# Recurrent attention and experts on one core: probabilities first on VectorE, idle products, a unit's scores split, loads in another order, two units a slot later

## What is computed

```
for t in range(S):
    m_new = maximum(f[t] + m, i[t])
    C = exp(f[t] + m - m_new) * C + exp(i[t] - m_new) * outer(v[t], k[t])
    n = exp(f[t] + m - m_new) * n + exp(i[t] - m_new) * k[t]
    y[t] = sigmoid(o[t]) * (C @ q[t]) / maximum(abs(n . q[t]), 1)
x = y as (1536, 320);  p = domain_probs / sum(domain_probs)
out = sum over 4 experts e of p[:, e] * (relu(x @ w1[e]) @ w2[e])       # w1 320x1024, w2 1024x320
```

## Time and profile before

| | us |
|---|---|
| median of 3 runs | 417.99 |
| the three runs | 418.11, 417.26, 417.99 |
| the profiled execution | 418.08 |
| its span, first to last instruction | 416.4 |
| busy: TensorE / VectorE / ScalarE / GpSimd | 411.6 / 180.6 / 158.5 / 152.3 |

### The profile page before, as it was taken

How to read it: one execution, slowest core, us unless ns; L and a number is a source line. 1 busy time by engine, 2 the same in 40 slices (tenths; PEclk the granted TensorE clock), 3 DMA queues, 4 the chain that set the end, 5 groups by cost and what they waited for, 6 DMA issues and landing times.

```text
span 416.4 us, 7050 instructions
## 1 busy us (share of the span) xinstructions
PE 411.6 (99%) x2710; PEld 398.3 (96%) x2710; DVE 180.6 (43%) x372; ACT 158.5 (38%) x329; POOL 152.3 (37%) x189
## 2 busy tenths in 40 slices
PE   8999999999999999999999999999999999999997
PEld 8899999999999999999999999999999999999996
DVE  5875796646555556446223232323113132311313
ACT  4575477745355653514112431144211333211111
POOL 4865735595174925304011660065100453000000
PEclk9999999999999999999999999999999999999999
DMA  7999939678513845300000231024200000000101
GB/s 269 272 283 394 369 100 354 226 256 290 189 37 131 303 132 193 122 2 0 2 0 2 85 129 67 0 71 139 71 0 2 0 0 2 34 0 2 63 0 65
DMA packets 16899, 48.45 MB, mean 116 GB/s; under 512 B 1921, under 2 KB 8594, under 8 KB 15714
## 3 DMA queue, kind: packets, MB, share of 16 engines
q1 hardware_dynamic: 16290, 46.60, 31.9%
q10 hardware_dynamic: 576, 1.40, 1.0%
HBM read 45.94 MB, written 2.05 MB: 115 GB/s over the span
## 4 chain that ended last, share of the span: by engine, by line
PE 98%; DVE 1%; issue 0%; DVEq 0%
PE hid_ps L1076 42%; PE acc_ps L1095 37%; PE out_ps L1032 5%; PE score_ps L1095 3%; PE acc_ps L1076 2%; PE out_ps L1039 2%; PE score_ps L976 2%; PE add_ps L1011 1%; PE hid_ps L925 1%; PE score_ps L971 1%; PE acc_ps L1032 0%; PE out_ps L1051 0%; PE out_ps L1052 0%; PE out_ps L1053 0%; PE score_ps L989 0%
## 5 line engine op out<-in xcount | busy, mean ns | idle before, releaser
L810 DVE SCALAR_TENSOR_TENSOR h_lo<-hid_ps,h_hi 128x384 fp32r<-128x384 f32 (+2 forms) x120 | 68.0, 567 | 219.7 <-ACT h_hi L587 219.6
L587 ACT ACTIVATE h_hi<-hid_ps 128x384 fp32r<-128x384 f32 (+2 forms) x120 | 59.6, 497 | 231.9 <-PE hid_ps L1076 231.8
L1095 PE MATMUL acc_ps<-w_hi,h_hi 128*128 128x320 f32 x352 | 110.2, 313 | 0.0
L1095 PE MATMUL acc_ps<-w_hi,h_lo 128*128 128x320 f32 x352 | 108.8, 309 | 0.0
L1095 PE MATMUL acc_ps<-w_lo,h_hi 128*128 128x320 f32 x352 | 108.4, 308 | 0.0
L1076 PE MATMUL hid_ps<-xt_hi,w_hi 128*128 128x384 f32 (+2 forms) x360 | 104.1, 343 | 0.1
L1076 PE MATMUL hid_ps<-xt_hi,w_lo 128*128 128x384 f32 (+2 forms) x360 | 103.7, 342 | 0.0
L441 POOL TENSOR_TENSOR w_lo<-w_raw,w_hi 128x384 fp32r<-128x384 f32 x56 | 58.9, 1054 | 114.5 <-ACT w_hi L573 114.5
L1076 PEld LDWEIGHTS hid_ps<-xt_hi,w_lo 128*128 128x128 f32 x360 | 65.4, 189 | 4.3
L1095 PEld LDWEIGHTS acc_ps<-w_hi,h_hi 128*128 128x128 f32 x352 | 66.3, 188 | 1.3
L1095 PEld LDWEIGHTS acc_ps<-w_lo,h_hi 128*128 128x128 f32 x352 | 66.3, 188 | 1.3
(11 more groups left out here) (172 smaller groups left out, 371.9 us busy)
## 6 DMA issues: line engine op xcount, KB each, us to landing
w_raw<-in_w_b SPq DMA_DIRECT2D x27, 704.0 KB, 4.3
raw<-in_qk_s SPq DMA_DIRECT2D x8, 1024.0 KB
g_all<-g_dram SPq DMA_DIRECT2D x10, 512.0 KB, 6.1
kv<-in_kv_n SPq DMA_DIRECT2D x12, 352.0 KB, 5.9
q_pack<-in_q_p SPq DMA_DIRECT2D x10, 192.0 KB, 6.1
out_y<-y_acc SPq DMA_DIRECT2D x12, 160.0 KB, 1.8
carry<-g_dram SPq DMA_DIRECT2D x30, 60.0 KB
y_acc<-in_o_n SPq DMA_DIRECT2D x1, 1280.0 KB, 12.3
```

What stands on the lines that cost most here:

```text
L587: nc.scalar.activation(h_hi[:, M % RING, 0:cols], hid_bank(M)[:, 0:cols], ACT.Relu).then_inc(hid_hi, 1)
L810: nc.vector.scalar_tensor_tensor(h_lo[:, M % RING, 0:cols], hid_bank(M)[:, 0:cols], 0.0, h_hi[:, M % RING, 0:cols].bitcast(fp32), ALU.max, ...
L1095: last = nc.tensor.matmul(acc_ps[t][:, 0:DM], x, w, start=(f == 0 and i == 0), stop=(f == NF - 1 and i == 2))
```

## The change

- Start, VectorE: `unit_maxima` moves ahead of all `probs`; `unit_steps` comes over from GpSimd and stands with `gate_scan(1)` ahead of `gate_x(0)`. The copy of the first key weights goes to ScalarE (`first_keys`), and the turned keys go to `hid_ps[0]` instead of `acc_ps[2]`.
- Start, TensorE: `move_ends` and `move_starts` come ahead of exponents and scores, and `keep_clock(3)` comes ahead of `outputs(0)`. `outputs(1)` waits for `w_tok`, not for `key_tok`.
- Start, ScalarE: pair 3 is issued and block 2 is split between the two `xt_high`; the scores of unit 3 are issued and the gates of tiles 2 and 3 opened between `relu(0)` and `relu(1)`.
- `NS` goes from 4 to 3: the fourth unit's (k = 3) scores take the split form, with casts in slots 4 and 5 and subtractions in slots 5 and 6. Two pairs of memsets of `raw` are one pair, and the memset of `state`'s last rows is gone, as products now read 120 or 80 rows.
- SP's order: the gates' stores come first behind pairs 0 and 1, then scores, gates, queries and carry of unit 2, its values, pair 4, and gates, queries, values and carry of unit 3, then pairs 5 to 7.
- `T0[2]` goes from 2 to 3 and `T0[3]` from 6 to 7.

Left out below are buffer shapes, semaphore names, and the split of `copy_keys` in two.

```diff
...
 RAW_PAIRS = 4
-NS = 4
+NS = 3
 KA, Q_ODD = 64 + D, 2 * HALF * L
...
 N_PAIRS = N_BLOCKS // 2
-T0 = {2: 2, 3: 6, 4: 16, 5: 22, 6: 28, 7: 32, 8: 38, 9: 44, 10: 48, 11: 54}
+T0 = {2: 3, 3: 7, 4: 16, 5: 22, 6: 28, 7: 32, 8: 38, 9: 44, 10: 48, 11: 54}
 EARLY = 24
 DN_FIRST, DN_END = 0, 20
-CAST = {4: (11, 12), 5: (16, 17), 6: (23, 24), 7: (26, 29), 8: (33, 35), 9: (39, 41), 10: (42, 45), 11: (49, 50)}
-SUB = {4: (13, 14), 5: (18, 19), 6: (25, 27), 7: (29, 30), 8: (35, 37), 9: (41, 43), 10: (45, 46), 11: (51, 53)}
-OPEN_IN = {3: (2,), 13: (4,), 14: (6,), 17: (8,), 18: (10,)}
+CAST = {3: (4, 5), 4: (11, 12), 5: (16, 17), 6: (23, 24), 7: (26, 29), 8: (33, 35), 9: (39, 41), 10: (42, 45), 11: (49, 50)}
+SUB = {3: (5, 6), 4: (13, 14), 5: (18, 19), 6: (25, 27), 7: (29, 30), 8: (35, 37), 9: (41, 43), 10: (45, 46), 11: (51, 53)}
+OPEN_IN = {13: (4,), 14: (6,), 17: (8,), 18: (10,)}
 LATER_PAIRS = {12: 8, 14: 9, 16: 10}
...
         y_acc, w_raw = landing("y_acc", [L, NT, DM]), landing("w_raw", [128, 2 * RAW_PAIRS, WB])
-        state, fresh = sb("state", [128, B, GROUP * GROUP * DA]), sb("fresh", [KS, GROUP * GROUP * DA])
+        state, fresh = sb("state", [KS, B, GROUP * GROUP * DA]), sb("fresh", [KS, GROUP * GROUP * DA])
         early = y_acc[0:U1, 4:NT, :].rearrange("u n m -> u (n m)")
...
         def scores_in(k):
-            return 16 * (k // 2 + 1)
+            return 16 * sum(2 if u < NS else 1 for u in range(B + k % 2, k + 1, 2))
...
             load_pair(sp, 1)
-            reload_scores(2)
-            load_q(2)
             sp.wait_ge(gate_tiles[1]["ready"], 2)
...
             sp.dma_start(g_dram[1, NU:NU + 1, :], gate_tiles[1]["gg"][0:1, 1, :]).then_inc(gate_tiles[1]["stored"], 16)
-            load_q(3)
+            reload_scores(2)
             sp.wait_ge(gate_tiles[1]["stored"], 3 * 16)
             load_g(2)
+            load_q(2)
+            load_carry(2)
             sp.wait_ge(out_done, 1)
...
             load_kv(sp, 2)
-            load_carry(2)
-            load_pair(sp, 3)
+            load_pair(sp, 4)
             load_g(3)
-            reload_scores(3)
+            load_q(3)
             sp.wait_ge(out_done, 2)
...
             load_carry(3)
-            load_pair(sp, 4)
             load_pair(sp, 5)
...
                     reload_scores(5)
-                if (k := unit_at(M, -2)) is not None and NS <= k < NT - 2:
+                if (k := unit_at(M, -2)) is not None and NS < k < NT - 2:
                     reload_scores(k + 2)
...
             pool.wait_ge(ident_ready, 2)
-            nc.gpsimd.memset(apart[0:64, 1, Q_ODD:Q_ODD + HALF * L], 0.0).then_inc(apart_set[1], 1)
-            nc.gpsimd.memset(apart[64:KA, 1, 0:HALF * L], 0.0).then_inc(apart_set[1], 1)
-            pool.wait_ge(apart_set[1], 2)
             nc.gpsimd.memset(kw[:, :, DM:], 0.0).then_inc(pool_init, 1)
...
                 pool.wait_ge(pool_init, 3)
-                st = state[0:KS, kept(k), :].rearrange("p (g c) -> p g c", g=GROUP)
+                st = state[:, kept(k), :].rearrange("p (g c) -> p g c", g=GROUP)
                 nc.gpsimd.tensor_tensor(st, st, decay[:, k - B, :].unsqueeze(2).broadcast_to([KS, GROUP, GROUP * DA]),
...
                 pool.wait_ge(state_scaled, k - B + 1)
-                nc.gpsimd.tensor_tensor(state[0:KS, kept(k), :], state[0:KS, kept(k), :], fresh[:, :], ALU.add)\
+                nc.gpsimd.tensor_tensor(state[:, kept(k), :], state[:, kept(k), :], fresh[:, :], ALU.add)\
                     .then_inc(state_ready, 1)
-            def unit_steps():
-                gt = gate_tiles[1]
-                pool.wait_ge(m_ready, 1)
-                pool.wait_ge(local_ready, 3)
-                nc.gpsimd.tensor_tensor(gt["fm"][:, :], gt["w"][:, :], m_u[:, :], ALU.add).then_inc(unit_step, 1)
-                pool.wait_ge(unit_step, 1)
-                nc.gpsimd.tensor_scalar(gt["g"][:, :], gt["fm"][:, :], 0.0, None, ALU.min).then_inc(unit_step, 1)
-                nc.gpsimd.tensor_scalar(gt["j"][:, :], gt["fm"][:, :], 0.0, -1.0, ALU.max, ALU.mult).then_inc(unit_step, 1)
...
             causal(1, 1)
-            unit_steps()
             weigh_keys(0)
+            unit_sums()
             weigh_keys(1)
-            unit_sums()
             for w in range(FIRST):
...
+            def first_keys():
+                gt = gate_tiles[0]
+                act.wait_ge(gt["key_ps"], 1)
+                nc.scalar.activation(key_w[:, 0:U0], hid_ps[0][:, U0:2 * U0], ACT.Copy).then_inc(gt["key_tok"], 1)
             def decays(k, half):
...
                 wait_if(act, s_ready, 2 * (k - 2) + 2)
-                nc.scalar.activation(split_qk[:, kept(k), t, :, :], raw[:, kept(k), t, :, :], ACT.Copy)\
+                nc.scalar.activation(split_qk[:, kept(k), t, :, :], raw[0:KS, kept(k), t, :, :], ACT.Copy)\
                     .then_inc(cast_done, 1)
...
             split_high(1, None)
+            first_keys()
             act.dma_start(y_acc[:, 2:4, :], o_n[:, 2:4, :]).then_inc(o_in[1], 16)
...
             xt_high(0)
+            load_pair(act, 3)
+            split_high(2, None)
             xt_high(1)
-            split_high(2, None)
             split_high(3, None)
             relu(0)
+            load_scores(act, 3)
+            gate_open(2)
             relu(1)
...
             nc.vector.memset(ones[:, :], 1.0).then_inc(ones_set, 1)
-            nc.vector.memset(apart[0:64, 0, Q_ODD:Q_ODD + HALF * L], 0.0).then_inc(apart_set[0], 1)
-            nc.vector.memset(apart[64:KA, 0, 0:HALF * L], 0.0).then_inc(apart_set[0], 1)
-            nc.vector.memset(state[96:128, :, 0:H * DA], 0.0).then_inc(rows_set, 1)
+            nc.vector.memset(apart[0:64, 0, Q_ODD:Q_ODD + HALF * L], 0.0).then_inc(apart_set, 1)
+            nc.vector.memset(apart[64:KA, 0, 0:HALF * L], 0.0).then_inc(apart_set, 1)
             nc.vector.memset(g_parts[:, :].bitcast(fp32), 0.0).then_inc(parts_set, 1)
...
+            def unit_steps():
+                gt = gate_tiles[1]
+                dve.wait_ge(m_ready, 1)
+                dve.wait_ge(local_ready, 3)
+                nc.vector.tensor_tensor(gt["fm"][:, :], gt["w"][:, :], m_u[:, :], ALU.add).then_inc(unit_step, 1)
+                dve.wait_ge(unit_step, 1)
+                nc.vector.tensor_scalar(gt["g"][:, :], gt["fm"][:, :], 0.0, None, ALU.min).then_inc(unit_step, 1)
+                nc.vector.tensor_scalar(gt["j"][:, :], gt["fm"][:, :], 0.0, -1.0, ALU.max, ALU.mult).then_inc(unit_step, 1)
             local_maxima()
             unit_starts()
+            unit_maxima()
...
                 else:
-                    dve.wait_ge(rows_set, 1)
-                    target = state[0:KS, k, 0:H * DA]
+                    target = state[:, k, 0:H * DA]
                 nc.vector.tensor_tensor(target, add_bank.get(k, add_ps)[0:KS, 0:H * DA],
...
             probs(0, 1)
-            unit_maxima()
             probs(1, 0)
             probs(1, 1)
-            copy_keys(0, 0, U0, acc_ps[2])
+            unit_steps()
+            gate_scan(1)
             gate_x(0)
-            gate_scan(1)
             gate_x(1)
...
                 if k < NS:
-                    pe.wait_ge(apart_set[kept(k)], 2)
+                    pe.wait_ge(apart_set, 2)
                     for j in range(2):
...
                 elif k == 1:
-                    pe.wait_ge(gate_tiles[0]["key_tok"], 1)
+                    pe.wait_ge(gate_tiles[0]["w_tok"], 1)
                 elif k == B:
...
                     for g, (first, n) in enumerate(G_OF):
-                        last = nc.tensor.matmul(bank[:, first * DA:(first + n) * DA], q_pack[:, kept(k), g, :],
-                                                state[:, kept(k), first * DA:(first + n) * DA],
+                        last = nc.tensor.matmul(bank[:, first * DA:(first + n) * DA], q_pack[0:n * D, kept(k), g, :],
+                                                state[0:n * D, kept(k), first * DA:(first + n) * DA],
                                                 start=False, stop=True, skip_group_check=True)
...
             exponents_first(0, 1)
+            move_ends()
             exponents_first(1, 0)
             exponents_first(1, 1)
-            move_ends()
+            move_starts()
             first_scores(0)
-            move_starts()
             first_scores(1)
+            pe.wait_ge(m_begun, 1)
+            keep_clock(3)
             outputs(0)
...
             pe.wait_ge(g0["w_tok"], 1)
-            turn(g0, "key", acc_ps[2], U0, U0, "key_ps")
+            turn(g0, "key", hid_ps[0], U0, U0, "key_ps")
             outputs(1)
...
             additions(0)
+            pe.wait_ge(g0["key_tok"], 1)
             keep_clock(2)
```

More of the change, by code:

```diff
@@ L684, in copy_tokens, with later_keys @@
                 nc.vector.tensor_copy(w_tok[:, first:first + rows], bank[:, 0:rows]).then_inc(gt["w_tok"], 1)
-            def copy_keys(n, first, rows, bank):
-                gt = gate_tiles[n]
+            def later_keys():
+                gt = gate_tiles[1]
```

(2 more changed lines are left out.)

11 lines of the change are left out of this document (6 added, 5 removed).

## The result

| | before | after |
|---|---|---|
| median | 418.21 (9 executions, 417.26 to 418.80) | 421.55 (9 executions, 419.71 to 426.07) |
| the profiled execution | 418.08 | 421.39 |
| its span | 416.4 | 419.7 |
| its mean granted TensorE clock | 1.000 | 0.996 |

The ratio is 1.0079, interval 1.0063 to 1.0095: the changed kernel is slower by 0.8%, 3.3 us. 417.9 was forecast, 419.1 at most.

What follows compares the result with a forecast made beforehand. TensorE was taken to bound the kernel (98% of the chain). Terms -0.1 - 0.84 - 0.4 + 1.2 + 0.1 = -0.04 on the profiled 418.08 gave 418.0, taken as 417.9; range 416.6 to 419.1.

Steps and rivals of the forecast that it cites:

- Part 1: The start, up to `up(0)`: the rearranged order there was to give -0.1 us, between -0.3 and +0.5.
- Part 2: Unit 3's scores in split form: 0.44 us a half instead of 0.86, two halves giving -0.84, certain to 0.1.
- Part 3: Stalls in `up(6)` and `up(8)` from late weight pairs were to go with earlier loads: -0.4 us (0 to -0.4).
- Rival D: Start fails: ScalarE stands at `gate_open(2)`, or `outputs(0)` starts over 0.6 late; +0.5 to +0.9, 418.4 to 418.8, chance 0.07.
- I set no price or gain for the clock itself.: TensorE's granted clock: taken as full in all slices of the profile before, so counted at nothing.
- Part 4: Units 2 and 3 one slot later: new wait of 1.2 us at `down(8)`, +0.1 at `up(16)`, moving itself free.
- rival B: No wait at `down(8)`, or under 0.4, as `gate_x(2)` gets through early: 416.8, or 416.5; chance 0.22.
- the lower end given: Wait at `down(8)`: 0.8 instead of 1.2 if the hidden half or the gate ran quicker than the rows.
- The +0.1 at `up(16)`: `transpose_x(3)` in slot 13, one ahead of `up(16)`: TensorE waits +0.1 us for tile 3 (0 to +0.3).
- Rival C: VectorE comes late into slot 7, the wait at `down(8)` grows by 1.0: 419.0 to 419.4; chance 0.13.
- C's other sign: `scores(3, 0)` on TensorE may also wait for VectorE's second subtraction; no separate size given.
- A: The forecast, 417.9 (417.3 to 418.6): gains of scores and early weights are given back at `down(8)`; chance 0.58.

Runs made afterwards that it cites:

- e8: e9 without the three idle products ahead of `outputs(0)`: 417.62, ratio 0.9989 to the kernel before.
- e9: The changed kernel with pair 3 issued by SP directly behind pair 1, and `add_expert(0)` ahead of `gate_x(2)` in slot 7: 417.78, ratio 0.9991 to before.
- e11: e9 with unit 3's scores back in the apart form (`NS = 4`, load 416 KB and not 1024 KB): 418.35, ratio 0.9998 to before.
- e1: The changed kernel with unit 3's scores issued by SP behind unit 3's carry, not by ScalarE behind `relu(0)`: 425.61, ratio 1.0182 to before.
- e5: The changed kernel with pair 3 issued by SP directly behind pair 1, not on ScalarE's queue at 15.7: 418.43, ratio 1.0008 to before.
- e12: The kernel before with only pair 3 moved, issued by SP directly behind pair 1: 418.89, ratio 1.0018 to before.
- e6: The changed kernel with eight idle products behind `down(3)`, where TensorE waits anyway: 422.57, ratio 1.0117 to before.
- e4: The changed kernel with `add_expert(0)` ahead of `gate_x(2)` and `probs(3, 0)` in VectorE's slot 7: 420.98, ratio 1.0071 to before.
- e2: The changed kernel with pair 3 issued by SP behind unit 2's values, not by ScalarE: 422.95, ratio 1.0113 to before.
- e3: The changed kernel with unit 2's scores issued by SP directly behind pair 1, not between the gates' stores and read: 419.40, ratio 1.0031 to before.
- e10: e9 with TensorE's order of moves, exponents and first scores at the start as before the change: 418.29, ratio 0.9995 to before.
- e7: The kernel before with only units 2 and 3 a slot later (`T0` 3 and 7): 423.27, ratio 1.0118 to before.

## Why the prediction was wrong

- **Part 1, start -0.1 (-0.3 to +0.5).** Right: 12.05 against 12.00 once the idle products are taken out, `outputs(1)` without its wait, and e8 level. Its marks by the clock on the wall, "`up(0)` at 18.8 to 18.9", missed (18.13), as the length of the idle products differs by 0.9 from one execution to the next.
- **Part 2, -0.84.** Right by rows in after. Where TensorE doesn't lose time at `up(6)`, VectorE comes late with the second subtraction and 0.47 is left of the 0.84 (e9 against e11); the times don't tell the gain from nothing. That ScalarE's extra load had a place and a price was missed: issued late by SP (e1) it makes the kernel 4 us slower, issued together with the read of the gates (e8) it may hold that read.
- **Part 3, -0.4: the step that failed.** The stalls of the old order are gone, as said. The sentence behind it, "the gates of unit 2 (512 KB, landing 4 to 7 us after their issue at 19.5) come at 24 to 26 against a need at 26.3; that margin is the thin one", had the right place and the wrong input. The read takes 5.39 us, within 4 to 7. The issue at 19.5 was wrong: it fits the 2.4 us from store to read of the profile before, carried over, although the change puts 704 KB on the other queue 0.7 us ahead of the last store. It was 22.85. From there all follows: landing at 28.25, ScalarE's 2.57, TensorE's 2.1. Rival D named the wait ("ScalarE stands at `gate_open(2)` for the later-issued gates") but priced it at 0.5 to 0.9 and gave it 0.07. e5 moves that one load and comes to 418.43, 0.5 from the forecast. The gain on the two stalls (-0.4) is read from rows of after alone: e12, which was to have it by itself, is 0.7 slower than before by the medians, as the same wait for the gates came up in it.
- **"I set no price or gain for the clock itself."** A second term put at nothing, 1.6 us in the profiled execution. Before granted 1.0 all along, and the text took that as a given; what sets the fall off isn't shown (e6).
- **Part 4, +1.2 at down(8).** Right in mechanism and near in size (1.20 listed, 1.35 from start to start), against rival B, whose missing wait e4 gets by another order on VectorE. In e5 0.8 is listed, the lower end given, but not because the hidden half or the gate ran quicker: TensorE came later. The +0.1 at `up(16)` was 0.25, within 0 to +0.3.
- **Rival C (VectorE late)** didn't happen in after: VectorE waited 1.36 ahead of `hidden_low(9)`, but with the 3.7 us that TensorE lost from `up(6)` to `up(7)` to help it. In e5 it has no idle time there and is just in time (`hidden_low(9)` 1.65 behind `up(9)` in both), and C's other sign came true: `scores(3, 0)` waits for a second subtraction of 1.68. C's growth by 1.0 at `down(8)` is seen nowhere. Its time, 419.0 to 419.4, would have been nearer than the forecast, for a reason that wasn't there.
- The forecast's sum without the gates, -0.04, is borne out: e5 stands at 1.0008 (0.9993 to 1.0024) of before. That the change's own parts cancel, as A said, is shown by rows (0.84 and 0.4 against 1.35 and 0.25); in time the wait at `down(8)` is worth 0.65 (e9 against e5, which ran beside it), and the split's gain is within the spread. The split and the slots together with the eviction first (e9, 0.9991, and e8, 0.9989) are no faster than before by what these runs can tell.

Open: what sets off the fall of the clock at the start. The profiles show it in e2, e3 and e9, and single executions of after, e4, e5, e6 and e8 have the mean clock that goes with it (0.992 or less); all of these have `move_ends` and `move_starts` ahead. With the old order none of e10's eleven and e12's twelve has a mean under 0.999; of the 29 of before that ran beside e10 two have 0.996, at 418.54 and 419.01. But e11's twelve have the new order too and show none, so the order isn't shown to be the cause. Where the other two executions of e7 lost theirs isn't known either, as only one was profiled.

## What to carry to other kernels

When a store to DRAM is read back, list every transfer that is issued ahead of the store on any queue, and when the last of them lands: here the reader was issued close to that time, from 1.5 to 6.4 us behind the same stores. Then list what is issued beside the read. Before a large load is moved, ask which small round trip it now stands in front of, and put it well ahead or behind the read; well ahead helps only if nothing else is then still under way at the stores (in e12 it pushed the loads behind it there). And give an idle time of TensorE of one microsecond a chance of costing more than itself: in these profiles the granted clock fell behind some such gaps and not behind others.
